# A mixing layer and two feed-forward networks on one core: block 0 rearranged and the accumulator emptied in tile 14

## The chip, the cores and the metric

The kernel runs on one core of one Trainium2 chip. The metric is the device time of one execution in microseconds; lower is better. Times of a profile are counted from the first instruction of the profiled execution.

## What is computed

The input is x (2 x 4096 x 192) and, for each token, 8 heads of 7 logits. The reference, cut to what matters:

```python
w = softmax(weight_gen)                      # over the 7 taps, per token and head
out[b, s, h] = sum_k w[b, s, h, k] * x_pad[b, s + k, h]   # causal window of 7 tokens, heads of 24
xn = out / sqrt(mean(out * out) + 1e-6) * rms_g
y = (silu(xn @ w_gate) * (xn @ w_val)) @ w_out1           # 192 -> 1536 -> 192
h = y @ w_in
result = (h * sigmoid(1.702 * h)) @ w_out2                # 192 -> 2048 -> 192
```

Everything is float32. A product is made of three: a value is split into a rounded part (hi) and a remainder (lo), and hi*hi, lo*hi and hi*lo are summed.

## The kernel before

Each partition owns 64 tokens and takes four at a time, so a group is 512 tokens and there are 16 groups. Block i runs the first network on group i (12 tiles of 128 hidden columns, u = 0 to 11) and then the second network on group i - 1 (16 tiles, u = 12 to 27). Block 0 has tiles 0 to 11 only, block 16 has tiles 12 to 27 only. Blocks 0 to 14 also mix group i + 1.

A tile of the first network: TensorE makes gate and value in two PSUM banks of `up_ps`, ScalarE takes SiLU, VectorE multiplies (L733, the product), ScalarE rounds it to `h_hi` (L552), VectorE subtracts to get `h_lo` (L742). The down projection of tile u - 2 is interleaved with the up projection of tile u. So TensorE leads by up to two tiles. A tile of the second network has a GELU (L542) on ScalarE in place of SiLU and product. Matmuls run in two halves of 64 rows (`top`, L775, and `low`, L779).

The first network's result collects in two banks of the accumulator, `acc_main` and `acc_rest`. ScalarE copies the main part (`empty_main`, L507), VectorE the rest with a shift and a sum (`empty_y_rest`, L677 and L679), both at tile 15 (`EVAC_Y`) of the block. The second network's projection (`down2`) writes the same banks: its second tile waits for `main_out` and `rest_out`. It starts after the step of tiles 16 and 17.

Mixing of group i + 1 is spread over the tiles of block i by `MIX_SLOT`: softmax in tile 1, 13 multiplications and additions of taps in tiles 2 to 8, squares on ScalarE (`mix_square`), mean, power on GpSimd (`rms`, L395), scale. TensorE transposes the result (`turn_x`), ScalarE scales it (`scale_x`, L490 and L496), VectorE rounds and splits it (`split_x`). Group 0 has no block before it: its mixing is the head of the kernel. There the last of its four tokens is mixed by GpSimd and three by VectorE.

The 34 pieces of weights ("chunks") come over SyncE's queue into 8 places of 512 columns: 5 of `stage` and 3 lent by `y_f32` and `o_lo` for their first round only. Each piece is rounded (ScalarE for the first 10, `chunk_hi_half`; GpSimd for the others, L409) and its remainder is subtracted on GpSimd (L416, `split_chunk`). A place is loaded again after its last piece is split. SyncE issues in program order: logits, x (3 transfers), 8 pieces with the gains between them, then further pieces, x and logits of the next groups between them. GpSimd runs in program order as well: four pieces, `rms(0)`, pieces up to 19, `rms(1)`, the others.

## Time and profile before

| | |
|---|---|
| time, median of 3 runs | 1284.24 us (1282.88 to 1284.37) |
| the profiled execution | 1283.08 us |
| its span, first to last instruction | 1281.3 us |
| TensorE busy | 1218.1 us, 95% |
| VectorE busy | 789.9 us, 62% |
| ScalarE busy | 665.7 us, 52% |
| GpSimd busy | 99.6 us, 8% |

The time is 1.8 us above the span in the profiled execution. PE is TensorE's matmuls, DVE VectorE, ACT ScalarE, POOL GpSimd, SPq SyncE's queue of transfers. Matmuls of one engine overlap in the records, so a pause is best read from start to start.

### The profile page before, as it was taken

What the parts mean: (1) busy time and instruction counts of PE and PEld (TensorE: products, weight loads), DVE (VectorE), ACT (ScalarE), POOL (GpSimd) and SP (SyncE); (2) the same over time, 40 slices, a digit from 0 to 9 for tenths busy, and PEclk for the clock granted to TensorE, in tenths of its full rate; (3) what the DMA queues carried; (4) which work ended last, traced back from release to release, by engine and by line L of the source; (5) the groups of instructions that cost most, each with busy time, mean ns of one, the idle gap of its engine ahead of it and who ended that gap; (6) DMA issues with size and microseconds to landing.
All of it is one profiled execution on the core that took longest, in us unless ns stands there. A gap on an engine that the chain in (4) does not pass through costs nothing.

```text
span 1281.3 us, 28916 instructions
## 1 busy us (share of the span) xinstructions
PE 1218.1 (95%) x11968; PEld 1094.1 (85%) x11968; DVE 789.9 (62%) x1218; ACT 665.7 (52%) x1194; POOL 99.6 (8%) x108
## 2 busy tenths in 40 slices
PE   0889999999999999999999999999999999999998
PEld 0667898988989998888989999899988998889898
DVE  6879566484755748466484855748476474854532
ACT  2243555645555554555645455564655555454454
POOL 7874000000000000000000000000000000000000
PEclk9999999999999999999999999999999999999999
DMA  5331000000000001001000100001000000000000
GB/s 146 91 98 56 1 17 32 18 32 2 21 28 18 32 5 44 2 17 33 17 32 1 48 2 17 32 5 45 1 18 32 18 32 2 14 2 14 1 14 14
DMA packets 14625, 33.69 MB, mean 26 GB/s; under 512 B 1828, under 2 KB 7842, under 8 KB 14496
## 3 DMA queue, kind: packets, MB, share of 16 engines
q1 hardware_dynamic: 14496, 31.85, 7.8%
...
## 4 chain that ended last, share of the span: by engine, by line
PE 77%; ACT 7%; DVE 5%; issue 4%; ACTq 0%; DVEq 0%
PE up_ps L775 38%; PE acc L775 30%; PE acc L779 5%; PE up_ps L779 4%; ACT hidden L542 2%; ACT L542 1%; ACT h_hi L552 1%; DVE hidden L733 1%; DVE shifted L677 1%; DVE y_f L679 1%; ACT x_f L490 1%; ACT silu L536 1%; ACT x_f L496 1%; DVE mixed L629 0%; DVE h_lo L742 0%
## 5 line engine op out<-in xcount | busy, mean ns | idle before, releaser
L742 DVE TENSOR_TENSOR h_lo<-hidden,h_hi 128x512 fp32r<-128x512 f32 x448 | 313.2, 699 | 377.0 <-ACT h_hi L552 375.4
L552 ACT CAST h_hi<-hidden 128x512 fp32r<-128x512 f32 x448 | 278.3, 621 | 269.4 <-DVE hidden L733 261.8
L775 PE MATMUL acc<-out_w,h_hi 64*128 64x384 f32 x1024 | 302.7, 355 | 16.1 <-DVE y_f L679 15.1
L779 PE MATMUL acc<-out_w,h_hi 64*128 64x384 f32 x1024 | 302.6, 355 | 0.0
L542 ACT ACTIVATE hidden<-up_ps 128x512 f32<-128x512 f32 x256 | 152.6, 596 | 216.4 <-PE up_ps L779 216.2
L775 PE MATMUL up_ps<-x_hi,up_w 64*128 64x512 f32 x800 | 254.1, 397 | 2.0 <-DVE x_hi L648 1.8
L775 PE MATMUL acc<-out_w,h_lo 64*128 64x192 f32 x1024 | 255.0, 249 | 0.0
L779 PE MATMUL acc<-out_w,h_lo 64*128 64x192 f32 x1024 | 254.8, 249 | 0.0
L779 PE MATMUL up_ps<-x_hi,up_w 64*128 64x512 f32 x800 | 254.0, 397 | 0.0
L775 PEld LDWEIGHTS acc<-out_w,h_hi 64*128 64x128 f32 x1024 | 188.8, 184 | 23.3 <-issue 18.2
L775 PE MATMUL acc<-h_hi,out_w 64*128 64x512 f32 x576 | 196.2, 393 | 5.4 <-issue 1.6
L779 PE MATMUL acc<-h_hi,out_w 64*128 64x512 f32 x576 | 196.4, 394 | 0.0
L775 PEld LDWEIGHTS acc<-out_w,h_lo 64*128 64x128 f32 x1024 | 191.8, 187 | 2.8
L779 PEld LDWEIGHTS acc<-out_w,h_lo 64*128 64x128 f32 x1024 | 191.7, 187 | 0.0
L779 PEld LDWEIGHTS acc<-out_w,h_hi 64*128 64x128 f32 x1024 | 188.7, 184 | 0.0
L733 DVE TENSOR_TENSOR hidden<-silu,up_ps 128x512 f32<-128x512 f32 x192 | 131.4, 684 | 86.8 <-ACT silu L536 49.9
L775 PEld LDWEIGHTS up_ps<-x_hi,up_w 64*128 64x128 f32 x800 | 146.3, 188 | 24.0 <-POOL up_w L416 2.0
L775 PE MATMUL up_ps<-x_rest,up_w 64*128 64x512 f32 x400 | 160.0, 400 | 4.8 <-DVE x_rest L658 4.8
L779 PE MATMUL up_ps<-x_rest,up_w 64*128 64x512 f32 x400 | 161.4, 403 | 0.0
L775 PE MATMUL up_ps<-x_lo,up_w 64*128 64x512 f32 x400 | 159.5, 399 | 0.5 <-DVE x_lo L650 0.4
L779 PE MATMUL up_ps<-x_lo,up_w 64*128 64x512 f32 x400 | 157.8, 394 | 0.0
L536 ACT ACTIVATE silu<-up_ps 128x512 f32<-128x512 f32 x192 | 114.5, 596 | 82.1 <-PE up_ps L779 81.3
...
## 6 DMA issues: line engine op xcount, KB each, us to landing
...
stage<-in_moe_w_in_dram SPq DMA_DIRECT2D x4, 256.0 KB, 2.6
...
stage<-in_moe_w_val_dram SPq DMA_DIRECT2D x3, 256.0 KB, 3.8
...
```

Of the source, the lines that this page charges most:

```text
L490: nc.scalar.activation(x_f32[:, 0, :].rearrange("p (j h c) -> p j h c", j=STEP, h=2), turned[:, :, 0:2 * P].rearrange("p h (j c) -> p j h ...
L496: ins = nc.scalar.activation(to[:, :, b, :, :], turned[part, :, 2 * P:3 * P].rearrange("p h (a c) -> p a h c", a=2), ACT.Copy, scale=g_res ...
L536: nc.scalar.activation(silu[:, u % 2, :], up_ps[2 * (u % 2)][:, :], ACT.Silu).then_inc(silu_done, 1)
L542: nc.scalar.activation(hidden[:, u % 2, :], up_ps[u % 4][:, :], ACT.Gelu_apprx_sigmoid).then_inc(gelu_done, 1)
L552: nc.scalar.copy(h_hi[:, u % 4, :], hidden[:, u % 2, :]).then_inc(hi_ready, 1)
L677: nc.vector.tensor_copy(shifted[:, :], acc_rest[REST:P, :]).then_inc(shift_done, 1)
L679: nc.vector.tensor_tensor(y_f32[0:REST, 1, :], acc_rest[0:REST, :], shifted[:, :], ALU.add).then_inc(rest_out, 1)
L733: nc.vector.tensor_tensor(hidden[:, u % 2, :], silu[:, u % 2, :], up_ps[2 * (u % 2) + 1][:, :], ALU.mult).then_inc(prod_done, 1)
L742: nc.vector.tensor_tensor(h_lo[:, u % 4, :], hidden[:, u % 2, :], h_hi[:, u % 4, :].bitcast(F32), ALU.subtract).then_inc(lo_ready, 1)
L775: return nc.tensor.matmul(ps, w[TOP], data[TOP], start=start, stop=stop)
L779: return nc.tensor.matmul(ps, w[LOW], data[LOW], start=start, stop=stop)
```

## The change

The softmax steps get a counter of their own (`SOFT`, `soft`) so that they may run apart from the rest of the mixing.

- SyncE issues logits 0, x 0, the gains and logits 1, waits until x has landed, and only then issues pieces 0 to 10. `stage` has 8 places instead of 5, so 11 pieces can be loaded at first.
- VectorE mixes all four tokens of group 0; GpSimd waits until that mixing is over, splits piece 0, runs `rms(0)`, waits for it, splits pieces 1 to 17, runs `rms(1)` and waits for it, and splits the rest. It rounds nothing.
- ScalarE rounds all pieces: 0 to 6 ahead of the squares of group 0, then the exponential of group 1, pieces 7 to 10, and pieces 11 to 33 in block 0, two behind each tile's rounding.
- The softmax of group 1 is moved into the head, between the mixing of group 0 and its scale. Its taps start in tile 0 of block 0 (`MIX_SLOT_0`), squares are in tile 6, mean in 7, scale in 8.
- The rounding of x for groups 0 and 1 is on ScalarE (`hi_x`). Block 0 reads x from `y_hi`, `y_lo`, `y_rest` and `y_twin`, block 1 from the x buffers; so the second split doesn't wait for block 0.
- In blocks 1 to 15 `empty_y_rest` is in tile 14 (`EVAC_Y_REST`), and `empty_main` is ahead of tile 15's GELU instead of behind it.

The diff, changed lines only:

```diff
@@ -86,7 +86,8 @@
-MIX = ["max", "sub", "sum", "eps", "recip", "norm", "mul0", "mul1"]
+SOFT = ["max", "sub", "sum", "eps", "recip", "norm"]
+MIX = ["mul0", "mul1"]
@@ -94,6 +95,9 @@
+def soft_count(g, step):
+    return g * len(SOFT) + SOFT.index(step) + 1
@@ -102,9 +106,12 @@
-EVAC_O, EVAC_Y0, SQUARE, SPLIT_Y, X_T, EVAC_Y, LAST_Y, SPLIT_X = 1, 1, 8, 8, U1 - 1, U1 + 3, U1 + 4, U1 + 5
+MIX_SLOT_0 = {0: ["mul0", "mul1"], 1: ["mul2", "add1"], 2: ["mul3", "add2"], 3: ["mul4", "add3"],
+              4: ["mul5", "add4"], 5: ["mul6", "add5"], 6: ["add6"], 7: ["mean"], 8: ["scale"]}
+EVAC_O, EVAC_Y0, SQUARE_0, SQUARE, SPLIT_Y, X_T = 1, 1, 6, 8, 8, U1 - 1
+EVAC_Y_REST, EVAC_Y, LAST_Y, SPLIT_X = U1 + 2, U1 + 3, U1 + 4, U1 + 5
@@ -129,11 +136,10 @@
-SLOTS = 5
+SLOTS = 8
...
-ACT_HI = 10
-RMS0_AT = 4
-RMS1_AT = 20
+RMS0_AT = 1
+RMS1_AT = CHUNKS1
@@ -226,8 +232,7 @@
-    mix = sem("mix")
-    last_mix = sem("last_mix")
+    soft, mix = sem("soft"), sem("mix")
@@ -305,7 +310,7 @@
-                sp.wait_ge(mix, mix_count(g - 1, "sub"))
+                sp.wait_ge(soft, soft_count(g - 1, "sub"))
@@ -348,19 +353,17 @@
-        for n in range(4):
-            load_chunk(n)
...
-        for n in range(4, SLOTS + LENT):
-            load_chunk(n)
...
-        for n in range(SLOTS + LENT, ACT_HI):
+        sp.wait_ge(x_in, x_count(0))
+        for n in range(SLOTS + LENT):
...
-        for n in range(ACT_HI, CHUNKS1 + SLOTS):
+        for n in range(SLOTS + LENT, CHUNKS1 + SLOTS):
@@ -395,20 +398,12 @@
-        def split_chunk(n, hi_here):
+        def split_chunk(n):
...
-            if hi_here:
-                pool.wait_ge(staged[place_of(n)], staged_count(n))
-                for hi, f, _, _, _ in parts:
-                    if hi is not None:
-                        last = nc.gpsimd.tensor_copy(hi, f)
-                last.then_inc(chunk_hi, 1)
@@ -420,32 +415,19 @@
-        last_token = mixed[:, STEP - 1:STEP, :]
-        taps = [out_sb[:, 0:1, :], out_sb[:, 1:2, :]]
-        pool.wait_ge(x_in, x_count(0))
-        pool.wait_ge(halo_ready, B)
-        pool.wait_ge(mix, mix_count(0, "norm"))
-        nc.gpsimd.tensor_tensor(*tap_product(last_token, 0, STEP - 1, STEP), ALU.mult).then_inc(last_mix, 1)
-        for k in range(1, TAPS):
-            if k > 2:
-                pool.wait_ge(last_mix, 2 * (k - 2) + 1)
-            nc.gpsimd.tensor_tensor(*tap_product(taps[k % 2], k, STEP - 1, STEP), ALU.mult).then_inc(last_mix, 1)
-            pool.wait_ge(last_mix, 2 * k)
-            nc.gpsimd.tensor_tensor(last_token, last_token, taps[k % 2],
-                                    ALU.add).then_inc(last_mix, 1)
+        pool.wait_ge(mix, mix_count(0, f"add{TAPS - 1}"))
...
-            split_chunk(n, False)
+            split_chunk(n)
...
+        pool.wait_ge(rstd, 1)
...
-            split_chunk(n, n >= ACT_HI)
+            split_chunk(n)
...
+        pool.wait_ge(rstd, 2)
...
-            split_chunk(n, True)
+            split_chunk(n)
@@ -463,7 +445,7 @@
-            act.wait_ge(mix, mix_count(g, "sub"))
+            act.wait_ge(soft, soft_count(g, "sub"))
@@ -475,9 +457,6 @@
-                if g == 0 and j == STEP - 1:
-                    act.wait_ge(last_mix, 2 * TAPS - 1)
@@ -498,6 +477,15 @@
+        def hi_x(g):
+            hi, rest, twin = (x_hi, x_rest, x_twin) if g else (y_hi, y_rest, y_twin)
+            act.wait_ge(x_scaled, g * 2 + 1)
+            nc.scalar.copy(hi[:, :], x_f32[:, 0, :]).then_inc(x_hi_ready, 1)
+            act.wait_ge(x_scaled, g * 2 + 2)
+            nc.scalar.copy(twin[REST:P, :], x_f32[0:REST, 1, :])
+            nc.scalar.copy(rest[0:REST, :], x_f32[0:REST, 1, :]).then_inc(x_hi_ready, 1)
@@ -518,7 +506,7 @@
-            if mixing:
+            if mixing and i:
@@ -536,33 +524,39 @@
+                    if i < GROUPS and u == EVAC_Y:
+                        empty_main(i)
...
-                if 0 < i < GROUPS and u == EVAC_Y:
-                    empty_main(i)
...
-                if mixing and u == SQUARE:
+                if i == 0:
+                    for n in range(SLOTS + LENT + 2 * u, min(SLOTS + LENT + 2 * u + 2, len(chunks))):
+                        chunk_hi_half(n)
+                if mixing and u == (SQUARE if i else SQUARE_0):
...
+                if i == 0 and u == X_T:
+                    hi_x(1)
...
-        for n in range(SLOTS + LENT):
+        for n in range(SLOTS + LENT - 4):
...
-        for n in range(SLOTS + LENT, ACT_HI):
+        mix_exp(1)
+        for n in range(SLOTS + LENT - 4, SLOTS + LENT):
...
+        hi_x(0)
@@ -582,38 +576,36 @@
-            if not (g == 0 and step == MIX[0]):
+            if step in MIX and not (g == 0 and step == MIX[0]):
...
+            if step in SOFT and not (g == 0 and step == SOFT[0]):
+                dve.wait_ge(soft, soft_count(g, step) - 1)
...
-                if g:
-                    dve.wait_ge(mix, mix_count(g - 1, MIX[-1]))
...
-                dve.wait_ge(mix, mix_count(g, "max"))
+                if g:
+                    dve.wait_ge(mix, mix_count(g - 1, f"mul{TAPS - 1}"))
...
-                dve.wait_ge(mix, mix_count(g, "sum"))
...
-                dve.wait_ge(mix, mix_count(g, "eps"))
...
-                dve.wait_ge(mix, mix_count(g, "recip"))
...
-                toks = STEP - 1 if g == 0 else STEP
...
-                    dve.wait_ge(mix, mix_count(g, "norm"))
+                    dve.wait_ge(soft, soft_count(g, "norm"))
@@ -621,12 +613,11 @@
-                ins = nc.vector.tensor_tensor(*tap_product(to[:, 0:toks, :], k, 0, toks), ALU.mult)
+                ins = nc.vector.tensor_tensor(*tap_product(to, k, 0, STEP), ALU.mult)
...
-                toks = slice(0, STEP - 1 if g == 0 else STEP)
...
-                ins = nc.vector.tensor_tensor(mixed[:, toks, :], mixed[:, toks, :], tap_at(k)[:, toks, :], ALU.add)
+                ins = nc.vector.tensor_tensor(mixed[:, :, :], mixed[:, :, :], tap_at(k), ALU.add)
@@ -638,34 +629,37 @@
-            ins.then_inc(mix, 1)
-        def split_main(g, f32, hi, lo, hi_sem, ready):
+            ins.then_inc(soft if step in SOFT else mix, 1)
+        def split_main(g, f32, hi, lo, hi_sem, ready, hi_made=False):
...
-            nc.vector.tensor_copy(hi[:, :], f32[:, 0, :]).then_inc(hi_sem, 1)
+            if not hi_made:
+                nc.vector.tensor_copy(hi[:, :], f32[:, 0, :]).then_inc(hi_sem, 1)
...
-        def split_rest(g, f32, rest, twin, hi_sem, ready):
-            nc.vector.tensor_copy(rest[0:REST, :], f32[0:REST, 1, :]).then_inc(hi_sem, 1)
-            nc.vector.tensor_copy(twin[REST:P, :], f32[0:REST, 1, :])
+        def split_rest(g, f32, rest, twin, hi_sem, ready, hi_made=False):
+            if not hi_made:
+                nc.vector.tensor_copy(rest[0:REST, :], f32[0:REST, 1, :]).then_inc(hi_sem, 1)
+                nc.vector.tensor_copy(twin[REST:P, :], f32[0:REST, 1, :])
...
-            if g:
+            if g > 1:
...
+            hi, lo, rest, twin = (x_hi, x_lo, x_rest, x_twin) if g else (y_hi, y_lo, y_rest, y_twin)
...
-            split_main(g, x_f32, x_hi, x_lo, x_hi_ready, x_ready)
+            split_main(g, x_f32, hi, lo, x_hi_ready, x_ready, g < 2)
...
-            split_rest(g, x_f32, x_rest, x_twin, x_hi_ready, x_ready)
+            split_rest(g, x_f32, rest, twin, x_hi_ready, x_ready, g < 2)
@@ -700,8 +694,7 @@
-            if g:
-                dve.wait_ge(up_done, unit_at(i - 1, UNITS))
+            dve.wait_ge(up_done, unit_at(i - 1, UNITS) if g else U1)
@@ -710,7 +703,7 @@
-            if mixing and i != 1:
+            if mixing and i > 1:
@@ -721,7 +714,7 @@
-                if 0 < i < GROUPS and u == EVAC_Y:
+                if 0 < i < GROUPS and u == EVAC_Y_REST:
@@ -732,7 +725,7 @@
-                steps = MIX_SLOT.get(u, []) if mixing else []
+                steps = (MIX_SLOT if i else MIX_SLOT_0).get(u, []) if mixing else []
@@ -760,8 +753,16 @@
-        for step in MIX:
+        for step in SOFT:
...
+        for step in MIX[:-2]:
+            mix_step(0, step)
+        mix_step(1, "max")
+        mix_step(1, "sub")
+        mix_step(0, "mean")
+        for step in SOFT[2:]:
+            mix_step(1, step)
+        mix_step(0, "scale")
@@ -780,11 +781,12 @@
-            x = (x_hi, x_lo, x_rest, x_twin)
+            x, y = (x_hi, x_lo, x_rest, x_twin), (y_hi, y_lo, y_rest, y_twin)
...
-                return up_ps[2 * (p % 2)], up_ps[2 * (p % 2) + 1], p, U1 + p, x
+                return up_ps[2 * (p % 2)], up_ps[2 * (p % 2) + 1], p, U1 + p, x if i else y
...
-            y = x if i == GROUPS else (y_hi, y_lo, y_rest, y_twin)
+            if i == GROUPS:
+                y = x
...
```

## Rows read from the trace of the kernel before

**Rows 1.** List of waits, TensorE, whole span: total us, times, longest us.

```profile
PE acc L775 <- DVE y_f L679: 16.1, 16, 1.1
```

**Rows 2.** Timeline, block 7: start, us, engine, line, what [idle before <-releaser].

```profile
522.06 0.69 DVE L742 TENSOR_TENSOR h_lo<-hidden,h_hi 128x512 fp32r<-128x512 f32 x1 [0.46 <-ACT h_hi L552]
...
522.08 0.39 PE L779 MATMUL acc<-h_lo,out_w 64*128 64x512 f32 x1
...
523.57 0.58 ACT L507 COPY y_f<-acc 128x512 f32<-128x512 f32 x1
...
523.93 0.69 DVE L677 COPY shifted<-acc 64x512 f32<-64x512 f32 x1
523.97 0.36 PE L775 MATMUL acc<-out_w,h_hi 64*128 64x384 f32 x1
...
524.17 0.25 PE L775 MATMUL acc<-out_w,h_lo 64*128 64x192 f32 x1
...
524.66 0.68 DVE L679 TENSOR_TENSOR y_f<-acc,shifted 64x512 f32<-64x512 f32 x1
...
525.49 0.41 PE L775 MATMUL acc<-out_w,h_hi 64*128 64x384 f32 x1 [1.06 <-DVE y_f L679]
```

**Rows 3.** Timeline, block 15, TensorE after the same emptying.

```profile
1211.03 0.41 PE L775 MATMUL acc<-out_w,h_hi 64*128 64x384 f32 x1 [0.24 <-DVE y_f L679]
```

**Rows 4.** Windows: A:B length, busy us by engine, PEclk, DMA share, GB/s.

```profile
2.00:9.10 7.10, 0.00 (x0) 0.00 (x0) 3.16 (x8) 0.40 (x2) 0.00 (x0) 1.00 0.93 240
```

**Rows 5.** Timeline of the head.

```profile
9.13 1.13 DVE L624 TENSOR_TENSOR mixed<-x_win,probs 128x576 f32<-128x576 f32 x1 [2.70 <-DMA x_win<-in_x_dram]
...
22.65 0.36 ACT L481 ACTIVATE normed_all<-mixed 128x192 f32<-128x192 f32 x1 [5.96 <-DVE mixed L629]
...
24.24 0.86 DVE L632 TENSOR_SCALAR rms_stat<-rms_stat 128x4 f32<-128x4 f32 x1 [1.63 <-ACT normed_all L481]
...
27.84 1.02 POOL L395 TENSOR_TENSOR rms_stat<-rms_stat,neg_half 128x4 f32<-128x4 f32 x1
...
28.96 1.14 DVE L638 TENSOR_TENSOR normed_all<-mixed,rms_stat 128x512 f32<-128x512 f32 x1 [3.85 <-POOL rms_stat L395]
...
30.75 0.36 PE L1016 MATMUL acc<-ident,normed_all 64*128 64x64 f32 x1 [30.75 <-DVE normed_all L639]
...
32.34 0.94 ACT L496 ACTIVATE x_f<-acc,g_rest 64x256 f32<-64x256 f32 x2
...
38.45 0.79 PE L775 MATMUL up_ps<-x_rest,up_w 64*128 64x512 f32 x1 [2.62 <-DVE x_rest L658]
```

**Rows 6.** Timeline, block 0: products of tiles 0, 2, 7, 8; second x.

```profile
43.69 0.69 DVE L733 TENSOR_TENSOR hidden<-silu,up_ps 128x512 f32<-128x512 f32 x1 [4.38 <-PE up_ps L779]
...
50.07 0.68 DVE L733 TENSOR_TENSOR hidden<-silu,up_ps 128x512 f32<-128x512 f32 x1
...
71.31 0.68 DVE L733 TENSOR_TENSOR hidden<-silu,up_ps 128x512 f32<-128x512 f32 x1
...
74.25 0.68 DVE L733 TENSOR_TENSOR hidden<-silu,up_ps 128x512 f32<-128x512 f32 x1
...
91.87 0.79 PE L775 MATMUL up_ps<-x_rest,up_w 64*128 64x512 f32 x1 [2.19 <-DVE x_rest L658]
```

**Rows 7.** Groups by shape, VectorE, from 111 us: busy us, mean ns.

```profile
L629 DVE TENSOR_TENSOR mixed<-mixed,tap 128x768 f32<-128x768 f32 x56 | 53.2, 950 | 0.0
```

**Rows 8.** The page's groups of instructions and DMA issues.

```profile
L552 ACT CAST h_hi<-hidden 128x512 fp32r<-128x512 f32 x448 | 278.3, 621 | 269.4 <-DVE hidden L733 261.8
...
stage<-in_moe_w_in_dram SPq DMA_DIRECT2D x4, 256.0 KB, 2.6
```

**Rows 9.** Lines 416 and 409, GpSimd: duration ns min/median/max.

```profile
L416 POOL TENSOR_TENSOR up_w<-stage,up_w x9: 1262/1594/1890, 22.0 to 101.4; 128x512 fp32r<-128x512 f32 x9
...
L409 POOL CAST up_w<-stage x12: 611/784/1227, 46.8 to 102.8; 128x512 fp32r<-128x512 f32 x12
```

**Rows 10.** Windows, columns as in rows 4: after the second x.

```profile
91.87:97.60 5.73, 5.73 (x28) 4.45 (x30) 0.14 (x1) 0.60 (x1) 5.28 (x7) 0.50 0.40 125
```

## The prediction

> **What bounds the kernel now.** I first read the list of what TensorE waited for over the whole span. TensorE is busy almost throughout, so only its own gaps can be won. One wait repeats: the projection of the second network waits for the vector instruction that finishes emptying the accumulator, 16 times, 16.1 us in all [rows 1]. Then I read one block in order of time [rows 2]. After tile 13's low part (522.06) VectorE computes tile 14's low part, and only at 523.93 and 524.66 empties `acc_rest`, though TensorE wrote it last in a matmul begun at 522.08. TensorE's last matmul before the wait begins at 524.17 and the next at 525.49. Fourteen blocks (1 to 14) show this to within 0.01 us; block 15, without mixing, idles only 0.24 us [rows 3]; the sixteenth wait is block 0's accumulator, emptied in block 1, which the change leaves.
>
> The second place is the head. TensorE can't begin in earnest until the first x is scaled, rounded and split, at 38.45 us [rows 5]. Block 0 then runs at VectorE's pace, not TensorE's: from tile 2 to tile 7 the products start 4.25 us apart (50.07 to 71.31), and only 2.94 us apart once GpSimd is idle (71.31 to 74.25) [rows 6]. The second x releases TensorE at 91.87 [rows 6].
>
> **Emptying in tile 14, the large part.** `empty_y_rest` moves ahead of tile 14's low part on VectorE. It can start at 522.67: tile 13's low part started at 522.06, and a following independent instruction starts 0.61 us later (start to start of what VectorE does without a wait: 0.69 less an overlap of 0.08). The matmul begun at 522.08 lasts 0.39 us, so `acc_rest` is ready then. The pair of instructions ends 1.26 us sooner (523.93 - 522.67), at 524.08 in place of 525.34. TensorE restarted 0.15 us after that end, so its release comes at 524.23. Undelayed, TensorE would go on by pairs: the first matmul of the last pair began at 523.97, the second at 524.17, and one pair with the next overlaps to about 0.29 us a pair, so the next is due at 524.26. So 525.49 - 524.26 = 1.23 us of each stall goes, and I count 1.22 us: 14 x 1.22 = 17.1 us, and 0.2 us in block 15.
>
> What is late next? `acc_main`: its copy on ScalarE stood at 523.57 [rows 2]; moved ahead of tile 15's GELU it takes the place at 523.1 but waits for the last matmul of `acc_main`, three matmuls of 0.235 us behind that of 522.08, over at 523.2. It ends by 523.9, ahead of 524.26. Behind the waiting copy stand tile 15's GELU and rounding, some 0.5 us later than now; TensorE wants that GELU for its next step about 2 us later. Behind the vector pair stands tile 14's low part, 0.8 us later, which no one needs before the projection of tiles 14 and 15, over 4 us on. These delays are covered; the cover ends at 2 us. Bounds for the part: 0 (some other wait stands there) to 14 x 1.28 = 17.9 us; by the row nearest, 17.1.
>
> **x alone on the queue.** From 2.0 to 9.1 us the DMA moved 240 GB/s, or 1.70 MB [rows 4], of which x (951 KB) and the logits (112 KB) are 1.09 MB. Alone they need 4.5 us: x lands at 6.5 instead of 9.13 [rows 5]. The softmax ends at 6.43 anyway: VectorE had idled 2.70 us when x came [rows 5]. Bounds 6.5 and 9.1 (if x's short rows and not the neighbours set its time); I take 7.0. The weights start 5 us later and their 1.7 MB for the first seven pieces land, at that rate, near 16: before the squares need ScalarE.
>
> **Mixing all on VectorE.** 13 instructions took 9.13 to 22.65, 1.04 us each, on 576 elements beside GpSimd. On 768 elements alone one takes 0.950 us [rows 7], with 0.035 us between dependent ones 0.985: 12.8 us. Mixing ends at 19.8. GpSimd waits for that, so its subtractions no longer disturb. The squares take as before 1.6 us (22.65 to 24.24): mean at 21.4. GpSimd now has only piece 0 ahead of the power and is done with it; power 1.02 us [rows 5], ready at 22.9. But the softmax of group 1 stands ahead of `scale`: exponential and four steps, about 0.4 us each, end at 23.5, later than the power. Scale to transposes is 1.79 us (28.96 to 30.75): transposes at 25.4 instead of 30.75.
>
> **Roundings on ScalarE.** From the transposes to the end of the scalings 2.53 us (32.34 + 0.94 - 30.75): 28.0. Three roundings at 0.62 us [rows 8] (the 64-row ones are not in the trace; 0.62 for 128 rows is the nearest, and bounds are 0.4 and 0.62): 29.8. The last low part on VectorE takes 0.69 us alone, up to twice that beside GpSimd: 30.5 to 31.3, I take 31.1. So TensorE starts 7.3 us sooner than at 38.45, and tile 0's product, 5.24 us behind (43.69 - 38.45) [rows 5, 6], stands at 36.3.
>
> **Block 0.** Mixing starts in tile 0, the rounding of weight pieces 11 to 33 moves from GpSimd to ScalarE, two a tile, and GpSimd only subtracts. Price of disturbance: in the 21.2 us of rows 6 VectorE lost 21.2 - 5 x 2.94 = 6.5 us, while GpSimd rounded and subtracted about six pieces of 0.61 + 1.26 us [rows 9], 11.5 us of work; so 0.55 us lost per microsecond of GpSimd's work. Pieces 11 to 17 are 7.5 us of subtraction (four at 1.26, and three at 0.8, estimated by their fewer columns), 4.1 us lost. Tiles 0 to 4 take 5 x 2.94 + 4.1 = 18.8 us: tile 5's product at 55.1. From here ScalarE's round sets the pace: SiLU (taken at a rounding's 0.62), wait for the product 0.69, rounding 0.62, two pieces 1.24: 3.2 us. Tile 6 at 58.3; tile 7 also has the squares of 1.5 us before it, 63.0.
>
> Here comes a **new wait**. GpSimd computes rms(1) after piece 17, so it stands until tile 7's mean. The slot of piece 26 is piece 18's, still unsplit, and ScalarE rounds piece 26 in tile 7. From product 7: mean 0.8, power 1.02, subtraction 1.26, transfer 2.6 [rows 8], rounding 0.62, SiLU 0.62, semaphores 0.2: 7.1 us. Product 8 at 70.1. Three rounds of 3.3 us: product 11 at 80.0. Then product and rounding 1.3, a piece 0.6, scalings 1.5, three roundings 1.9, low part 0.7 to 1.4: second x ready at 86.3, against 91.87. Of 7.3 us won at the start 5.6 are left. The x buffers are free sooner by the second set, which saves nothing here: the scalings come last. Bounds of the head: +2 (x at 9.1, disturbance half as dear again) to +10.
>
> TensorE's clock: the stretch from 91.87 to 97.60 was granted 1.2 GHz, half of 2.4 [rows 10], after TensorE had idled 2.19 us for the second x [rows 6]. The start at 31.1 and the second x at 86.3 follow longer idleness, so I keep both slow stretches. A third can follow the wait at piece 26; TensorE isn't the bound there, so 0 to 2 us.
>
> **Sum.** 17.1 + 0.2 + 5.6 = 22.9 us. The profiled execution took 1283.08 us, its span 1281.3; it would be 1260.2. The median of the runs, 1284.24, becomes 1261.3; I say 1261.
>
> **A rule to weigh.** VectorE beside GpSimd: a 128x512 subtraction on GpSimd took from 1.26 to 1.89 us [rows 9] and VectorE lost 0.55 us per microsecond of it. The Trainium skill (SBUF — State Buffer, section Who interferes with whom) says that a vector instruction with two SBUF inputs and a GpSimd instruction reading SBUF exclude each other for a whole instruction. By that rule each microsecond of GpSimd's would cost one: the sum would lose 3.4 us more. The trace agrees only in part.
>
> **Rivals.**
> Full exclusion in block 0, as a mechanism of this kernel: 7.5 us lost instead of 4.1, so 1264.7. For it: subtractions alone, without roundings between, leave VectorE fewer openings. Against: the 0.55 of the rows. 0.12.
> Half the stall stays: the copy of `acc_main`, or a semaphore that comes 0.6 us later than I place it, releases TensorE. Then 14 x 0.6 are lost: 1269.7. Against: block 15, where ScalarE is early, shows 0.24 us. 0.11.
> The head wins nothing: x lands at 9.1 and piece 26 costs more: 1266.9. 0.08.
> Piece 26 costs nothing, because TensorE's lead of two tiles covers it: 3.8 us better, 1257.5. 0.08.
> Slower: pieces 26 to 33 wait for each other in turn, each with 1.26 + 2.6 + 0.62 = 4.5 us, and TensorE stands for seven more such rounds, 32 us: 1293. It decides when each piece waits for the one just before it. Against: each slot's predecessor is eight pieces back, rounded already, so the trips overlap. 0.02.
> The change does not do what it says (x no sooner, wait unmoved) is within 0.2%: 0.01.
>
> **How the numbers follow.** My case has 0.58 and its own bounds give 1256 to 1266. The range 1254 to 1269 takes in both head bounds, full exclusion and an idle head, and leaves the half stall out. A measurement of this kernel tells about 0.2% from no change; all cases but two are faster by more: 0.97, same 0.01, slower 0.02.
>
> **What would show it.** TensorE's list of waits has 14 fewer on the emptying, and the matmul after the emptying follows the one before it at once, 1.2 us sooner in each block. Transposes of x at 25.4, first full run at 31.1, tile 0's product at 36.3, ScalarE idle for about 4 us in tile 7 of block 0 for a transfer, second x near 86. I am wrong if the wait list shows `acc_main`'s copy or GELU in the place of the old wait, or if VectorE's steps between tiles 0 and 4 are far from 4 us.

## The result: 1261.7 us against 1283.8 us

The changed kernel takes 1261.67 us (median of four runs, 1261.61 to 1262.76); the kernel before took 1283.75 us in the same comparison. The ratio is 0.983, 95% interval 0.9813 to 0.9848. The forecast was 1261. The profiled execution took 1261.61 us with a span of 1259.8, so the span fell by 21.5 us.

TensorE's list of waits (total us, times, longest us), lines that answer to [rows 1]. The wait for the emptying is left once, in block 1 for block 0's accumulator; the other fifteen are gone. The longest behind the head is new: TensorE waits 3.8 us for a SiLU.

```profile
PE up_ps L776 <- ACT silu L524: 3.8, 1, 3.8
PE up_ps L776 <- ACT y_hi L484: 2.4, 1, 2.4
PE acc L776 <- POOL pair_lo L411: 1.4, 1, 1.4
...
PE acc L776 <- DVE y_f L673: 0.9, 1, 0.9
```

The same place of block 7 as in [rows 2], in order of time. The vector pair now starts 0.72 us behind tile 13's low part (1.87 us before), TensorE's last matmul ahead of the projection's second tile starts at 513.60 and the next at 513.76, 0.16 us apart instead of 1.32.

```profile
511.49 0.69 DVE L735 TENSOR_TENSOR h_lo<-hidden,h_hi 128x512 fp32r<-128x512 f32 x1 [0.46 <-ACT h_hi L539]
511.50 0.39 PE L776 MATMUL up_ps<-y_lo,up_w 64*128 64x512 f32 x1
...
512.21 0.69 DVE L671 COPY shifted<-acc 64x512 f32<-64x512 f32 x1
...
512.69 0.59 ACT L495 COPY y_f<-acc 128x512 f32<-128x512 f32 x1
...
512.94 0.68 DVE L673 TENSOR_TENSOR y_f<-acc,shifted 64x512 f32<-64x512 f32 x1
...
513.60 0.25 PE L776 MATMUL acc<-out_w,h_lo 64*128 64x192 f32 x1
...
513.76 0.41 PE L776 MATMUL acc<-out_w,h_hi 64*128 64x384 f32 x1
```

The head, answering to [rows 5]. The last multiplication of taps ends at 21.2; then come the subtraction of the softmax of group 1, the mean, GpSimd's first piece behind the power, the normalising, the two scalings, the transposes, ScalarE's scaling, and TensorE's first unbroken run.

```profile
8.22 0.96 DVE L616 TENSOR_TENSOR mixed<-x_win,probs 128x768 f32<-128x768 f32 x1 [2.07 <-DMA x_win<-in_x_dram]
...
21.49 1.27 DVE L592 TENSOR_TENSOR probs<-logits,head_stat 128x224 f32<-128x224 f32 x1
...
22.79 0.17 DVE L623 TENSOR_SCALAR rms_stat<-rms_stat 128x4 f32<-128x4 f32 x1
...
24.20 1.27 POOL L411 TENSOR_TENSOR pair_lo<-stage,up_w 64x512 fp32r<-64x512 f32 x1
24.30 1.41 DVE L601 TENSOR_TENSOR probs<-probs,head_stat 128x224 f32<-128x224 f32 x1
...
25.64 1.74 DVE L629 TENSOR_TENSOR normed_all<-mixed,rms_stat 128x512 f32<-128x512 f32 x1
...
27.31 1.48 DVE L630 TENSOR_TENSOR normed_all<-mixed,rms_stat 128x256 f32<-128x256 f32 x1
...
28.84 0.37 PE L1018 MATMUL acc<-ident,normed_all 64*128 64x64 f32 x1 [28.84 <-DVE normed_all L630]
...
30.44 0.94 ACT L475 ACTIVATE x_f<-acc,g_rest 64x256 f32<-64x256 f32 x2
...
34.63 0.79 PE L776 MATMUL up_ps<-y_rest,up_w 64*128 64x512 f32 x1 [0.84 <-DVE y_rest L651]
```

Block 0, answering to [rows 6]: VectorE's products of tiles 0, 5, 7, 8 and 11, then ScalarE's rounding of piece 26, then TensorE as the second x arrives.

```profile
40.23 0.69 DVE L726 TENSOR_TENSOR hidden<-silu,up_ps 128x512 f32<-128x512 f32 x1 [5.66 <-PE up_ps L780]
...
60.58 0.67 DVE L726 TENSOR_TENSOR hidden<-silu,up_ps 128x512 f32<-128x512 f32 x1
...
67.69 0.69 DVE L726 TENSOR_TENSOR hidden<-silu,up_ps 128x512 f32<-128x512 f32 x1 [2.03 <-ACT silu L524]
...
75.04 0.69 DVE L726 TENSOR_TENSOR hidden<-silu,up_ps 128x512 f32<-128x512 f32 x1 [5.28 <-ACT silu L524]
...
84.44 0.67 DVE L726 TENSOR_TENSOR hidden<-silu,up_ps 128x512 f32<-128x512 f32 x1
```

```profile
73.90 0.62 ACT L444 CAST up_w<-stage 128x512 fp32r<-128x512 f32 x1 [4.44 <-DMA stage<-in_moe_w_in_dram]
```

```profile
90.70 0.50 PE L776 MATMUL up_ps<-x_rest,up_w 64*128 64x512 f32 x1 [0.64 <-DVE x_rest L651]
```

Windows (length, busy us of PE, PEld, DVE, ACT and POOL, granted clock, DMA share, GB/s), answering to [rows 10]. The slow stretch is no longer behind the second x but behind the wait for piece 26.

```profile
75.30:78.80 3.50, 3.50 (x18) 3.15 (x20) 3.50 (x5) 2.05 (x4) 3.26 (x4) 0.52 0.61 184
90.70:97.00 6.30, 5.88 (x48) 4.43 (x48) 2.38 (x4) 4.28 (x7) 1.82 (x2) 1.00 0.00 0
```

### The profile page after: what moved, and what is told of

The parts are those of the page before. It is cut to its first block, busy times and chain, and to the rows that moved or that the text cites. A ratio compares the mean times of both kernels' runs of the same rounds, so it can differ in the third digit from the quotient of the medians.

```text
span 1259.8 us, 28858 instructions
## 1 busy us (share of the span) xinstructions
PE 1215.3 (96%) x11968; PEld 1059.8 (84%) x11968; DVE 781.2 (62%) x1212; ACT 684.3 (54%) x1228; POOL 65.5 (5%) x67
## 4 chain that ended last, share of the span: by engine, by line
PE 93%; DVE 3%; issue 1%; ACT 1%; DMA 1%; POOL 0%; SPq 0%; DVEq 0%; ACTq 0%; POOLq 0%
PE up_ps L776 49%; PE acc L776 37%; PE acc L780 3%; PE up_ps L780 3%; DVE mixed L620 1%; DVE tap L616 1%; DMA x_win<-in_x_dram 0%; DVE hidden L726 0%; PE acc L1018 0%; DVE normed_all L616 0%; DMA stage<-in_moe_w_in_dram 0%; DVE h_lo L735 0%; DVE mixed L616 0%; DVE normed_all L629 0%; PE acc L1022 0%
## 5 line engine op out<-in xcount | busy, mean ns | idle before, releaser
L780 PE MATMUL up_ps<-x_hi,up_w 64*128 64x512 f32 x752 | 236.8, 394 | 0.0
L776 PE MATMUL up_ps<-x_hi,up_w 64*128 64x512 f32 x752 | 236.3, 394 | 0.1
L776 PE MATMUL up_ps<-y_hi,up_w 64*128 64x512 f32 x528 | 171.1, 404 | 6.5 <-ACT silu L524 3.8
L780 PE MATMUL up_ps<-y_hi,up_w 64*128 64x512 f32 x528 | 167.6, 397 | 0.0
L776 PEld LDWEIGHTS up_ps<-x_hi,up_w 64*128 64x128 f32 x752 | 135.7, 186 | 27.5 <-issue 0.6
L776 PE MATMUL acc<-h_lo,out_w 64*128 64x512 f32 x384 | 151.8, 395 | 0.0
L780 PE MATMUL acc<-h_lo,out_w 64*128 64x512 f32 x384 | 150.9, 393 | 0.0
```

Source lines behind the costliest of these rows:

```text
L776: return nc.tensor.matmul(ps, w[TOP], data[TOP], start=start, stop=stop)
L780: return nc.tensor.matmul(ps, w[LOW], data[LOW], start=start, stop=stop)
```

## Where the 21.5 us come from

The span divides at two places that both traces have: the release of TensorE by the second x, and the matmul that follows the emptying in each block.

| stretch | before | after | won |
|---|---|---|---|
| start to second x | 91.87 | 90.70 | 1.2 |
| second x to the emptying's last instruction in block 1 | 51.24 | 46.50 | 4.7, of which 1.16 is block 1's own stall: 3.6 |
| emptying of blocks 1 to 14: 14 stalls | 1.32 us from start to start | 0.16 | 16.2 |
| block 15 (from the emptying of block 14) | 75.09 | 74.55 | 0.5 |

All experiments below are compared by these places. The first multiplication, the transposes and so on are starts, in us; "slow" is TensorE at 1.2 GHz, from and for how long. Left out are a slow stretch at the end and one at the start that every kernel has: TensorE's matmuls of 512 columns last 0.62 us up to 41 us in the changed kernel (43 us before) and 0.39 us from there on. Three kernels have no unbroken first run, because TensorE waits for subtractions in it. e2, e5, e8 and e9 rest on one execution each, e1, e3, e4, e6, e7, e10, e11 and e12 on four to nine.

| kernel | first mult. | transposes | first run | product 0 | 5 | 7 | 8 | 11 | second x | emptying, block 1 | slow | span |
|---|---|---|---|---|---|---|---|---|---|---|---|---|
| before | 9.13 | 30.75 | 38.45 | 43.69 | 62.97 | 71.31 | 74.25 | 84.66 | 91.87 | 143.11 | 90.8, 6.8 | 1281.3 |
| after | 8.22 | 28.84 | 34.63 | 40.23 | 60.58 | 67.69 | 75.04 | 84.44 | 90.70 | 137.20 | 75.2, 3.4 | 1259.8 |
| e1_emptying_only | 9.40 | 31.03 | 38.74 | 44.29 | 63.23 | 71.57 | 74.50 | 84.92 | 92.25 | 142.38 | 84.9, 10.2 | 1265.0 |
| e2_rest_only | 9.45 | 31.07 | 38.77 | 43.48 | 62.81 | 70.99 | 74.48 | 84.90 | 92.10 | 142.22 | 86.5, 10.2 | 1264.9 |
| e3_head_only | 7.85 | 28.47 | 34.26 | 39.86 | 60.22 | 67.34 | 74.66 | 84.69 | 91.64 | 140.62 | 74.1, 6.8; 91.2, 3.4 | 1278.8 |
| e4_rms1_late | 8.85 | 29.47 | 35.26 | 40.46 | 62.93 | 71.08 | 73.89 | 83.11 | 89.38 | 135.88 | none | 1258.5 |
| e5_x_truly_alone | 7.58 | 28.20 | 33.98 | 39.58 | 59.93 | 67.05 | 74.12 | 83.79 | 90.08 | 136.56 | 74.1, 3.4 | 1259.4 |
| e6_scale_undisturbed | 8.57 | 26.04 | | 36.42 | 58.22 | 65.33 | 72.41 | 82.10 | 88.37 | 134.85 | 72.6, 3.4 | 1257.6 |
| e7_rms1_20 | 8.32 | 28.94 | 34.72 | 40.32 | 62.78 | 69.89 | 72.69 | 82.95 | 89.22 | 137.16 | 89.0, 3.4 | 1259.9 |
| e8_round_on_vector | 7.70 | 28.33 | 36.98 | 42.58 | 62.92 | 70.04 | 77.12 | 86.80 | 95.41 | 144.32 | 77.1, 3.4; 94.2, 6.8 | 1267.3 |
| e9_second_x_waits | 8.35 | 28.98 | 34.75 | 40.35 | 60.72 | 67.83 | 74.88 | 84.61 | 90.88 | 137.37 | 75.4, 3.4 | 1260.1 |
| e10_three_together | 7.68 | 25.15 | | 36.47 | 59.48 | 67.63 | 70.44 | 79.65 | 85.93 | 132.42 | none | 1255.1 |
| e11_gpsimd_rounds | 8.60 | 29.22 | 34.99 | 40.15 | 61.36 | 67.88 | 69.86 | 78.81 | 86.43 | 136.55 | 87.2, 3.4 | 1259.2 |
| e12_last_eight_on_gpsimd | 8.18 | 25.65 | | 36.27 | 57.92 | 65.03 | 67.31 | 76.69 | 82.84 | 131.37 | 83.0, 3.4 | 1254.0 |

## The experiments

### The two parts apart

The emptying alone, in the kernel before:

```diff
+                        if i < GROUPS and u == EVAC_Y:
+                            empty_main(i)
                         act.wait_ge(up_done, U + 1)
...
-                    if 0 < i < GROUPS and u == EVAC_Y:
-                        empty_main(i)
...
-                    if 0 < i < GROUPS and u == EVAC_Y:
+                    if 0 < i < GROUPS and u == EVAC_Y - 1:
                         empty_y_rest(i)
```

> The kernel before with nothing changed but the place of the emptying: the copy of acc_main ahead of tile 15's GELU and the vector pair in tile 14, in blocks 1 to 15. If the emptying wins by itself what the changed kernel shows from block to block (period 75.15 us instead of 76.31), the span falls by 14 x 1.16 + 0.5 = 16.7 us, to 1264.6, and the time to 0.987 of before. If the shorter period needs the new block 0 as well, the period stays above 76 and the span within 2 us of 1281.

Measured: span 1265.0 us, period 75.15 us, 1266.73 us against 1283.10, ratio 0.987 (0.9854 to 0.9887). The span fell by 16.3 us, 0.4 short because the second x came 0.4 us later than in the kernel before, 0.3 us of it because x landed later in the head. TensorE was slow for 10.2 us around the second x instead of 6.8, but from there to the emptying of block 1 it took 50.1 us, as before without the stall. The emptying alone gives the whole steady part.

With only the vector pair moved, the second half of that diff:

```diff
-                    if 0 < i < GROUPS and u == EVAC_Y:
+                    if 0 < i < GROUPS and u == EVAC_Y - 1:
                         empty_y_rest(i)
```

> The kernel before with only the vector pair (acc_rest) moved to tile 14; acc_main is still copied behind tile 15's GELU. If the vector pair was the whole wait, the copy of acc_main (523.57 + 0.58 = 524.15) ends about when the pair now ends (524.08) and the period falls to 75.2 to 75.3: span 1265 to 1267. If acc_main's copy is late next, TensorE's list of waits shows it with 0.5 us or more a block and the span is 1272 or above.

Measured: span 1264.9 us, periods 75.15 to 75.19 us from block 2 on. The vector pair was the whole wait. The move of `acc_main`'s copy wins nothing that shows here.

The new block 0 alone, that is the changed kernel with the emptying back in its place:

```diff
-    EVAC_Y_REST, EVAC_Y, LAST_Y, SPLIT_X = U1 + 2, U1 + 3, U1 + 4, U1 + 5
+    EVAC_Y_REST, EVAC_Y, LAST_Y, SPLIT_X = U1 + 3, U1 + 3, U1 + 4, U1 + 5
...
-                        if i < GROUPS and u == EVAC_Y:
-                            empty_main(i)
                         act.wait_ge(up_done, U + 1)
...
                                              ACT.Gelu_apprx_sigmoid).then_inc(gelu_done, 1)
+                        if i < GROUPS and u == EVAC_Y:
+                            empty_main(i)
```

> The changed kernel with the emptying put back to tile 15 (both halves). If the two parts add up, block 0 and block 1 alone win 21.5 - 16.7 = 4.8 us: span 1276.5, period 76.3. If the new block 0 also changes the steady blocks, the span is below 1274.

Measured: span 1278.8 us, period 76.3 us, 1279.31 us against 1283.10, ratio 0.9972 (0.9962 to 0.9981). It won 2.5 us in the profile and 3.8 in the medians, not 4.8. From product 0 to product 8 it runs like the changed kernel; then it had slow stretches of 6.8 and 3.4 us, the second x came 0.9 us later, and block 1 took 1.3 us more besides the stall. With these 2.2 us the parts add up; the fastest of its nine executions has the 1276.5 us forecast as its span. The waits of TensorE for the emptying in this kernel, and then in e1_emptying_only:

```profile
PE acc L776 <- DVE y_f L673: 16.1, 16, 1.1
```

```profile
PE acc L775 <- DVE y_f L679: 1.8, 1, 1.8
```

### The wait for piece 26, and the clock

> The changed kernel with rms(1) behind piece 21 in place of piece 17, so that the slots of pieces 26 to 29 are free before GpSimd waits for the mean. ScalarE's wait of 4.4 us for piece 26 in tile 7 goes and product 8 comes 4.0 us sooner, the second x at about 86.7 instead of 90.7. Theory of the clock: TensorE then has no pause of 3.8 us in block 0, keeps 2.4 GHz there, and meets the slow stretch behind the second x instead, which costs about 2.6 us: the span falls by only 1.4 us, to 1258.4. Rival: the slow stretch isn't moved; the whole 4 us are won: 1255.8.

```diff
-    RMS1_AT = CHUNKS1
+    RMS1_AT = 22
```

Measured: span 1258.5 us, 1259.83 against 1283.10, ratio 0.9818 (0.9803 to 0.9833). The number is that of my theory of the clock, the reasons are not. The wait is gone (product 8 follows 2.81 us behind product 7, 7.35 before), but the second x is only 1.95 us sooner counted from the transposes (59.9 instead of 61.9). VectorE's products of tiles 4, 5, 6, 7 and 8 show why:

```profile
57.88 0.68 DVE L726 TENSOR_TENSOR hidden<-silu,up_ps 128x512 f32<-128x512 f32 x1
...
62.93 0.67 DVE L726 TENSOR_TENSOR hidden<-silu,up_ps 128x512 f32<-128x512 f32 x1
...
66.91 0.68 DVE L726 TENSOR_TENSOR hidden<-silu,up_ps 128x512 f32<-128x512 f32 x1
...
71.08 0.69 DVE L726 TENSOR_TENSOR hidden<-silu,up_ps 128x512 f32<-128x512 f32 x1 [2.03 <-ACT silu L524]
...
73.89 0.69 DVE L726 TENSOR_TENSOR hidden<-silu,up_ps 128x512 f32<-128x512 f32 x1 [0.74 <-ACT silu L524]
```

From tile 4 to 5 it takes 5.05 us and from 5 to 6 3.98, where the changed kernel takes 2.94 for each. The four pieces 18 to 21 that GpSimd subtracts in its former pause stretch VectorE's work: 3.1 us lost, of the 4.5 won in tile 7. Another 0.4 us of the 1.95 has nothing to do with the edit: TensorE reached 2.4 GHz 4.4 us behind its first run here and 6.5 in the changed kernel, and product 0 came 11.0 us behind the transposes instead of 11.4. And no slow stretch came at all:

```profile
89.40:97.00 7.60, 6.66 (x55) 5.19 (x57) 3.65 (x6) 4.51 (x8) 1.82 (x2) 1.00 0.00 0
```

A smaller step, `RMS1_AT = 20`:

> The changed kernel with rms(1) behind piece 19 (piece 17 in the changed kernel, piece 21 in the experiment before). There four more subtractions, 4.8 us of GpSimd's work, lengthened tiles 4 and 5 by 3.1 us while the wait of 4.1 us went. By that price two subtractions cost 1.8 us and the pause at tile 7 still goes nearly whole: second x 2.3 us sooner relative to the transposes (59.6 us behind them instead of 61.9). Rival: the slots of pieces 28 and 29 now make ScalarE wait in tile 8 instead, and the second x is no sooner than with piece 21 (59.9).

```diff
-    RMS1_AT = CHUNKS1
+    RMS1_AT = 20
```

Measured: the second x comes 60.3 us behind the transposes, so my 59.6 fell and the rival held. It is no sooner than with piece 21; counted from product 0 both kernels need 48.9 us. VectorE loses 2.1 us in tile 4 only, but ScalarE waits for a transfer in tile 8, and product 9 comes 4.37 us behind product 8 (3.34 with piece 21). Span 1259.9 us, 1260.21 against 1283.82, ratio 0.9819 (0.9804 to 0.9834). TensorE was at 1.2 GHz behind the second x in this run:

```profile
89.20:92.50 3.30, 3.28 (x16) 2.59 (x18) 0.00 (x0) 1.99 (x3) 2.55 (x3) 0.51 0.00 0
```

From the second x to the emptying of block 1 this kernel took 47.9 us, and the six that kept 2.4 GHz there took 46.5 each (after, e4, e5, e6, e9, e10). A stretch of 3.4 us costs 1.4 us. The kernel before, slow for 5.7 us after the release, took 51.24 less 1.16 of its stall, 50.1: 3.6 more, of which 2.6 are the clock by the spacing of matmuls (0.43 us slow, 0.235 fast). e8_round_on_vector, below, bears this out: slow for 5.6 us after the release, with GpSimd as idle as in the changed kernel, it took 48.9, 2.4 more. The rest, about 1 us, goes with GpSimd: it was busy 18.1 us of that stretch before and 2.8 after. That last share is read from the traces, not isolated.

### Why the head wins less than forecast

> The changed kernel with the gains and the logits of group 1 issued behind the wait for x, so that nothing but x and the first logits is on the queue. If these neighbours held x back, the first multiplication starts near 7.0 us, as I had predicted, instead of 8.2 (7.9 to 8.9 in the three profiles with this head). If x's own transfer and its completion take that long, it stays between 7.8 and 8.9 and the span stays within 1 us of 1259.8.

The gains and logits 1 are issued behind the wait for x, among the pieces:

```diff
-            sp.dma_start(g_main[:, :], g_v[0:P, :]).then_inc(g_in, 16)
-            for half in range(2):
-                sp.dma_start(g_rest[half * REST:(half + 1) * REST, :], g_v[P:D, :]).then_inc(g_in, 16)
-            load_logits(1)
             sp.wait_ge(x_in, x_count(0))
-            for n in range(SLOTS + LENT):
+            for n in range(2):
+                load_chunk(n)
+            load_logits(1)
+            for n in range(2, 7):
+                load_chunk(n)
+            sp.dma_start(g_main[:, :], g_v[0:P, :]).then_inc(g_in, 16)
+            for half in range(2):
+                sp.dma_start(g_rest[half * REST:(half + 1) * REST, :], g_v[P:D, :]).then_inc(g_in, 16)
+            for n in range(7, SLOTS + LENT):
                 load_chunk(n)
```

Windows of its head (columns as above):

```profile
2.00:7.00 5.00, 0.00 (x0) 0.00 (x0) 3.16 (x8) 0.40 (x2) 0.00 (x0) 1.00 0.66 213
7.00:7.58 0.58, 0.00 (x0) 0.00 (x0) 0.00 (x1) 0.00 (x0) 0.00 (x0) 1.00 0.00 0
```

The transfer is over before 7.0 and x is used at 7.58: between the two expectations. So 0.6 us at least lie between the last packet and the release, which my division of bytes by rate had left out. What the neighbours cost is not shown. In the eight profiles with the change's order on the queue the first multiplication starts at 7.70 to 8.85 (mean 8.3), in the three with nothing beside x at 7.58, 7.68 and 8.18 (mean 7.8): the two ranges overlap. The kernel before shows 9.13 and, in e1 and e2, 9.40 and 9.45. Span 1259.4.

> The changed kernel with GpSimd waiting for the scale of group 0 before it subtracts piece 1 (it waited for the power only). Theory: three vector instructions ahead of the transposes (normalising the softmax of group 1, 1.41 us, and the two scalings, 1.74 and 1.48) are stretched by GpSimd and take about 0.4, 0.7 and 0.5 alone, so the transposes come 2.8 us after the squares' mean plus its chain, about 2.9 us sooner relative to the first multiplication (17.7 us behind it instead of 20.6). GpSimd's pieces come 1.6 us later, which costs nothing if tile 0 doesn't wait for them: second x 2.9 us sooner. Rival: pieces 1 to 3 or 11 to 17 are then late, TensorE waits for a subtraction instead, and the second x comes less than 1 us sooner.

```diff
-            pool.wait_ge(rstd, 1)
+            pool.wait_ge(mix, mix_count(0, "scale"))
```

```profile
24.65 0.39 DVE L601 TENSOR_TENSOR probs<-probs,head_stat 128x224 f32<-128x224 f32 x1
24.96 0.69 DVE L629 TENSOR_TENSOR normed_all<-mixed,rms_stat 128x512 f32<-128x512 f32 x1
25.57 0.42 DVE L630 TENSOR_TENSOR normed_all<-mixed,rms_stat 128x256 f32<-128x256 f32 x1
```

Measured: the normalising and two scalings take 0.39, 0.69 and 0.42 us against 1.41, 1.74 and 1.48 with GpSimd beside them. Transposes 17.5 us behind the first multiplication (20.6), second x 79.8 behind it (82.5): 2.7 us sooner, against a forecast of 2.9. TensorE then waits 3.1 us for a subtraction in tile 0: the wait that the rival named is there, but not its price (second x less than 1 us sooner). Counted from the first multiplication product 0 is 4.2 us sooner than in the changed kernel and product 5 2.7: 1.5 us are lost again in tiles 0 to 4, and none behind them. Span 1257.6 us; 1259.78 against 1283.82, ratio 0.9815 (0.9799 to 0.9832).

> The changed kernel with x rounded by VectorE again, for groups 0 and 1, in the buffers of the change. Theory: ScalarE's roundings run beside VectorE's subtractions and are not stretched by GpSimd; from the transposes to TensorE's first unbroken run it took 7.70 us before and takes 5.79 now. Undone it is 7.6 to 7.8 again, and the second x, where 4.4 us became 2.8, loses another 1.5: it comes 65.3 us behind the transposes instead of 61.9. Rival: block 0's own waits take up the loss at its start, and the second x comes at most 63.5 us behind.

```diff
-            hi_x(0)
...
-                    if i == 0 and u == X_T:
-                        hi_x(1)
...
-                split_main(g, x_f32, hi, lo, x_hi_ready, x_ready, g < 2)
+                split_main(g, x_f32, hi, lo, x_hi_ready, x_ready)
...
-                split_rest(g, x_f32, rest, twin, x_hi_ready, x_ready, g < 2)
+                split_rest(g, x_f32, rest, twin, x_hi_ready, x_ready)
```

VectorE's instructions on the first x (low part, two roundings of 64 rows, last low part):

```profile
30.81 1.64 DVE L639 TENSOR_TENSOR y_lo<-x_f,y_hi 128x512 fp32r<-128x512 f32 x1
32.38 1.48 DVE L644 CAST y_rest<-x_f 64x512 fp32r<-64x512 f32 x1
33.89 1.37 DVE L646 CAST y_twin<-x_f 64x512 fp32r<-64x512 f32 x1
35.18 1.74 DVE L648 TENSOR_TENSOR y_rest<-x_f,y_rest 64x512 fp32r<-64x512 f32 x1
```

Measured: the first run starts 8.65 us behind the transposes (5.79), the second x 67.1 (61.9). The roundings on ScalarE are worth 5.2 us at the second x, more than my theory's 3.4, because all five of VectorE's instructions are stretched. Undisturbed in later blocks, VectorE's roundings take 0.41 to 0.42 us, less than ScalarE's 0.62; beside GpSimd the three took 0.71, 1.48 and 1.37. The last subtraction took 1.74 us here and 1.18 in the changed kernel. With a slow stretch of 6.8 us around the second x the span is 1267.3 us. Its second x stands at 95.41, behind the 91.87 of the kernel before: in this run the rest of the new block 0 doesn't pay for itself up to there.

> The changed kernel, but ScalarE and VectorE wait before they write the second x until TensorE has read block 0's x for the last time, as if both shared one set of buffers. My claim that the second set saves nothing here: no wait shows, the second x comes 61.9 us behind the transposes, as in the changed kernel. If the second set matters, it comes later by the length of that wait, 0.5 us or more.

```diff
                 hi, rest, twin = (x_hi, x_rest, x_twin) if g else (y_hi, y_rest, y_twin)
+                if g:
+                    act.wait_ge(up_done, U1)
...
-                if g > 1:
+                if g:
                     dve.wait_ge(up_done, unit_at(g - 1, U1))
```

Measured: 61.9 us behind the transposes, no wait, span 1260.1. The second set of buffers alone wins nothing.

> The changed kernel with GpSimd rounding pieces 11 to 33 again, while ScalarE does none of them in block 0. Theory: VectorE loses 0.6 us for each microsecond of GpSimd's work, and seven roundings of 0.61 us in tiles 0 to 4 cost it 2.5 us there; GpSimd's work also reaches into block 1. The second x comes 1 to 3 us later and the span is 1261 to 1264. Rival: ScalarE's two roundings a tile are themselves on the path from tile 5 on (VectorE waits for ScalarE there), so that freeing ScalarE wins them back and the span is 1259 or less.

```diff
+                if n >= SLOTS + LENT:
+                    pool.wait_ge(staged[place_of(n)], staged_count(n))
+                    for hi, f, _, _, _ in parts:
+                        if hi is not None:
+                            last = nc.gpsimd.tensor_copy(hi, f)
+                    last.then_inc(chunk_hi, 1)
                 pool.wait_ge(chunk_hi, n + 1)
...
-                    if i == 0:
-                        for n in range(SLOTS + LENT + 2 * u, min(SLOTS + LENT + 2 * u + 2, len(chunks))):
-                            chunk_hi_half(n)
```

Measured: my theory fell, and the rival's mechanism showed, though not its span of 1259 or less. The second x comes 57.2 us behind the transposes, 4.7 sooner than in the changed kernel, since ScalarE no longer waits for piece 26 and tile 8 follows 1.98 us behind tile 7. From product 0 to 5 it took 21.2 us against 20.35. But block 1 takes 50.1 us from the second x to the emptying instead of 46.5, with GpSimd busy until 106 us and one slow stretch. What is won in block 0 is lost in block 1: span 1259.2, 1260.20 against 1283.19, ratio 0.982 (0.9807 to 0.9834).

### Better versions

> The changed kernel with three of the edits above: nothing beside x on the queue, GpSimd's pieces behind the scale of group 0, rms(1) behind piece 21. If they add up (0.6 us by the first, 2.7 by the second, 2.0 by the third, each as seen at the second x), the second x comes near 85.4 us and, with TensorE at 2.4 GHz behind it, the emptying of block 1 at 131.9: span 1254.5. If TensorE falls to 1.2 GHz behind the second x, as with rms(1) behind piece 19, add 1.5 to 2.6 us. If the gains exclude each other, because GpSimd's later pieces now lie in tiles 0 to 5 with four more subtractions, the span is 1257 or above without a slow stretch.

The edit of e5_x_truly_alone, and:

```diff
-            pool.wait_ge(rstd, 1)
+            pool.wait_ge(mix, mix_count(0, "scale"))
...
-    RMS1_AT = CHUNKS1
+    RMS1_AT = 22
```

Measured: second x 85.93, emptying of block 1 at 132.42, span 1255.1 us. 1256.75 us against 1283.19, ratio 0.9795 (0.9782 to 0.9809). Forecast were 85.4, 131.9 and 1254.5. Counted from the first multiplication the second x is 4.2 us sooner than in the changed kernel; e4 and e6 had won 2.0 and 2.7 that way. The three add up to within 0.6 us.

> The changed kernel with nothing beside x on the queue, GpSimd's pieces behind the scale of group 0, rms(1) behind piece 17 as in the change, but pieces 26 to 33 rounded by GpSimd instead of ScalarE. Nobody on the path waits for piece 26 any more, and GpSimd still rests in tiles 4 to 7. Theory: tile 7 and tiles 8 to 11 go as with GpSimd rounding all (product 7 to product 11 in 10.9 us instead of 16.8), second x near 82.2 us; GpSimd works on to about 94 us, costing block 1 about 2 us: emptying of block 1 near 130.7 us, span 1253.4, or 1255 with TensorE at 1.2 GHz for a while behind the second x. Rival: what is won in block 0 is lost in block 1, as there, and the span is 1255.1 or more, no better than the three edits together.

The edits of e5_x_truly_alone and e6_scale_undisturbed, and:

```diff
+    ACT_HI = 26
...
+                if n >= ACT_HI:
+                    pool.wait_ge(staged[place_of(n)], staged_count(n))
+                    for hi, f, _, _, _ in parts:
+                        if hi is not None:
+                            last = nc.gpsimd.tensor_copy(hi, f)
+                    last.then_inc(chunk_hi, 1)
                 pool.wait_ge(chunk_hi, n + 1)
...
-                        for n in range(SLOTS + LENT + 2 * u, min(SLOTS + LENT + 2 * u + 2, len(chunks))):
+                        for n in range(SLOTS + LENT + 2 * u, min(SLOTS + LENT + 2 * u + 2, ACT_HI)):
```

Measured: second x 82.84, emptying of block 1 at 131.37, span 1254.0 us in the profiled execution, which had a slow stretch behind the second x; 1254.18 us (median of five, 1253.73 to 1255.74) against 1283.24, ratio 0.9773 (0.976 to 0.9787). It is the fastest here: its slowest execution is below the fastest of e10_three_together (1256.22). The rival fell and the theory held, 0.6 us short at the second x, because product 7 to 11 took 11.7 us and not 10.9. Block 1 took 48.5 us instead of 46.5, 1.4 of it by the clock if a stretch of 3.4 us costs here what it cost in e7. In tile 7 ScalarE rounds piece 25 (66.28) and goes straight to the SiLU:

```profile
66.28 0.51 ACT L455 CAST out_w<-stage 128x384 fp32r<-128x384 f32 x1
66.69 0.59 ACT L535 ACTIVATE silu<-up_ps 128x512 f32<-128x512 f32 x1
68.03 0.62 ACT L550 CAST h_hi<-hidden 128x512 fp32r<-128x512 f32 x1 [0.75 <-DVE hidden L737]
```

## Why the prediction was right, and where it was not

**The emptying (17.3 us forecast, 16.7 measured).** The mechanism was as written, and e1 and e2 isolate it. The size was off by 0.07 us a block: I let the vector pair start 0.61 us behind tile 13's low part, and it starts 0.72 behind. Block 15 gave 0.5 us instead of 0.2. `acc_main` is late next by nothing: its copy waits for the last matmul as I said (512.69) and ends ahead of the release. The rival of half the stall is refuted by the period of 75.15 us.

**x alone.** Step "4.5 us: x lands at 6.5, I take 7.0": it was 8.22. 0.6 us of the error lie between the last packet and the release (e5); how the rest divides between the neighbours and the swing from one execution to another stays open.

**Mixing on VectorE.** 0.985 us forecast, 0.99 measured (8.22 to 21.2 for 13).

**From mean to transposes.** Here the forecast of the head failed most: 20.6 us from the first multiplication to the transposes, where I had 18.4. I took "scale to transposes is 1.79 us" from a trace where GpSimd disturbed it little, and put the softmax of group 1 at 0.4 us a step. GpSimd starts its pieces at 24.2, and three vector instructions ahead of the transposes cost 4.6 us instead of 1.5. Transposes at 28.84 instead of 25.4, 1.2 us of it by x; e6 shows the cause of the rest by removing it (17.5 us instead of 20.6).

**Roundings.** 5.7 us forecast from transposes to the first run, 5.79 measured; 5.24 to the product, 5.6 measured. That distance follows the slow stretch at the start, which I took as unchanged: TensorE reached 2.4 GHz 4.5 us behind the first run before and 6.5 in the changed kernel; in e4 and e11, with 4.4 us, the product stands 5.2 us behind.

**Block 0.** From product 0 to 5 forecast 18.8, measured 20.35, in steps of 3.5, 6.1, 4.0, 3.7 and 2.9 us. Both factors were too small. GpSimd's pieces of `out_w`, two instructions of 256 columns each, take 1.15 us (37.13 to 38.28), not 0.8, so its work is 8.5 us and not 7.5; and VectorE lost 0.66 us per microsecond of it, not 0.55. The 0.55 came from a stretch with roundings between the subtractions. By e11 these seem to cost less: six subtractions of 7.4 us and six roundings of 3.7 us, undisturbed, went with 6.5 us lost from product 0 to 5, which leaves about 0.4 us per microsecond of rounding if the subtractions cost 0.66 there too. That is an estimate, not isolated. To product 7 26.7 forecast, 27.5 measured. The wait for piece 26 is there as worked out: 7.1 us forecast from product 7 to 8, 7.35 measured, ScalarE idle 4.44 us for the transfer. Then 9.9 forecast and 9.4 measured, and 6.3 and 6.26 to the second x. So the second x came at 90.70, not at 86.3: all 4.4 us were lost ahead of product 0 (3.9) and in the tiles (0.5). The 0.5 is a balance: 1.55 us too little for tiles 0 to 4 and 0.25 for the wait, against 0.8 and 0.5 too much for tiles 5 to 7 and 8 to 11.

**The clock.** "I keep both slow stretches" was right for the one at the start and wrong for the one behind the second x. The third one that I allowed behind piece 26 came, in every profile that has that wait, and where it was 3.4 us long the stretch behind the second x was fast, in all but e8. Together with GpSimd's absence in block 1 this won 3.6 us that I had priced at nothing. So the total is right (22.9 forecast, 21.5 in the span) because 4.4 us too much in block 0 and 0.6 in the emptying stand against 3.6 too little in block 1. For the head that is luck. Only the large part was right on its own.

**Full exclusion.** The rival had VectorE lose 7.5 us in tiles 0 to 4, my case 4.1. It lost 20.35 - 5 x 2.94 = 5.65 us beside seven subtractions that take 4 x 1.27 + 3 x 1.15 = 8.5 us undisturbed, 0.66 per microsecond: between the two. A single pair of instructions does show the exclusion. The softmax's subtraction for group 0, with GpSimd idle; then GpSimd's piece 0, piece 10 undisturbed, piece 11, and pieces 16 and 17:

```profile
3.82 0.39 DVE L592 TENSOR_TENSOR probs<-logits,head_stat 128x224 f32<-128x224 f32 x1
...
21.24 1.27 POOL L411 TENSOR_TENSOR up_w<-stage,up_w 128x512 fp32r<-128x512 f32 x1 [19.74 <-DVE mixed L620]
...
37.13 1.15 POOL L411 TENSOR_TENSOR out_w<-o_lo,out_w 128x256 fp32r<-128x256 f32 x2
42.22 1.91 POOL L411 TENSOR_TENSOR out_w<-stage,out_w 128x256 fp32r<-128x256 f32 x2 [3.94 <-ACT out_w L444]
...
53.24 4.81 POOL L411 TENSOR_TENSOR out_w<-stage,out_w 128x256 fp32r<-128x256 f32 x4
```

Piece 0 ran from 21.24 to 22.51 in its usual 1.27 us; the subtraction of the softmax, issued 0.25 us behind it, ended at 22.76 and took 1.27 us instead of 0.39. Begun when GpSimd was done it would have ended at 22.51 + 0.39 = 22.90. That is the exclusion for whole instructions of which the Trainium skill tells (SBUF — State Buffer, section Who interferes with whom), within 0.15 us. What I had wrong is who pays. The same seven pieces took GpSimd 12.65 us in the tiles instead of 8.5, so it lost 4.1 us beside VectorE's 5.65. Here the two engines shared the loss, and a microsecond of the one didn't cost the other a whole one; VectorE's products, which read PSUM, kept their 0.67 to 0.69 us throughout. That is a reading of this trace, not tested by itself.
